# A delta rule and two expert layers: weight groups of the second layer split in another order, a second output buffer, waits by accumulator

## The reference

```python
for t in range(S):
    y[:, :, t] = einsum('bhd,bhde->bhe', q[:, :, t], state)
    v_old = einsum('bhde,bhd->bhe', state, k_n[:, :, t])
    state = state + beta_t * outer(k_n[:, :, t], v_t - v_old)
h = x @ w_in            # first layer
g = where(h >= 1, h, where(h <= -1, 0, (h + 1)**2 / 4))
x = g @ w_out
h = x @ w_in2           # second layer
r = maximum(h, 0.0)
out = (r * r) @ w_out2
```

## Time and profile before

| | |
|---|---|
| median of three runs | 1002.56 us (1001.31 to 1002.76) |
| profiled execution | 1000.11 us, its span 998.0 us |
| mean granted clock of TensorE | 0.975 of full speed |
| PE (TensorE matmul) busy | 951.9 us, 95% |
| VectorE (DVE), ScalarE (ACT), GpSimd (POOL) busy | 669.7, 455.0, 171.4 us |
| longest waits of PE | 14.9, 5.1, and two of 1.9 us |

### The profile page before, as it was taken

The page is one execution under the profiler, slowest core; times in us unless marked ns, Lnnn a source line. Parts: engine busy times, 40 slices in busy tenths (PEclk is TensorE's granted clock), DMA queues, the critical chain, the costliest instruction groups (busy, mean ns, idle before and its releaser), DMA issues. The chain is left out here.

```text
span 998.0 us, 23043 instructions
## 1 busy us (share of the span) xinstructions
PE 951.9 (95%) x9448; PEld 768.6 (77%) x9448; DVE 669.7 (67%) x1566; ACT 455.0 (46%) x768; POOL 171.4 (17%) x165
## 2 busy tenths in 40 slices
PE   7899999999999999999999965999999999999997
PEld 6688788778777877787788854788877888878885
DVE  7789789787888888797545424655656565646553
ACT  6667443554454445435445433433543334533333
POOL 5810000000000000000025855560223001400000
PEclk7799999999999999999999996999999999999999
DMA  7252140122012101200030321210011000010001
GB/s 252 82 171 65 59 129 34 34 71 73 18 34 88 56 17 34 60 33 2 12 133 5 107 68 38 75 63 2 0 60 68 1 1 1 22 41 1 1 1 64
DMA packets 31015, 51.71 MB, mean 52 GB/s; under 512 B 2496, under 2 KB 19904, under 8 KB 30912
## 3 DMA queue, kind: packets, MB, share of 16 engines
q1 hardware_dynamic: 30912, 50.24, 15.2%
HBM read 40.80 MB, written 9.44 MB: 50 GB/s over the span
## 5 line engine op out<-in xcount | busy, mean ns | idle before, releaser
L1555 PE MATMUL psum<-x_high,w 128*128 128x512 f32 x528 | 193.1, 396 | 21.5 <-DVE act_g L2038 16.4
L1546 PE MATMUL psum<-g_hi,w 128*128 128x512 f32 x576 | 197.6, 399 | 0.0
L1527 PE MATMUL psum<-x_hi,w 128*128 128x512 f32 x576 | 197.3, 398 | 0.0
L2003 DVE TENSOR_TENSOR act_g<-act_g 128x512 f32<-128x512 f32 x96 | 74.4, 775 | 97.6 <-ACT act_g L1126 68.2
L1555 PEld LDWEIGHTS psum<-x_high,w 128*128 128x128 f32 x528 | 100.6, 191 | 45.7 <-issue 22.8
L1546 PEld LDWEIGHTS psum<-g_hi,w 128*128 128x128 f32 x576 | 108.4, 188 | 26.3 <-issue 2.0
L1527 PEld LDWEIGHTS psum<-x_hi,w 128*128 128x128 f32 x576 | 108.0, 188 | 26.4
L1546 PE MATMUL psum<-g_lo,w 128*128 128x512 f32 x288 | 112.5, 391 | 0.0
L1527 PE MATMUL psum<-x_lo,w 128*128 128x512 f32 x288 | 111.9, 390 | 0.0
L1034 ACT ACTIVATE act_g<-act_g,half 128x512 f32<-128x512 f32 x86 | 62.1, 723 | 106.1 <-DVE act_g L1955 105.6
L1625 PE MATMUL psum<-quad_hi,w 128*128 128x512 f32 x288 | 105.8, 395 | 3.8 <-ACT y_out L1060 3.8
(11 more groups left out here) (187 smaller groups left out, 1448.9 us busy)
## 6 DMA issues: line engine op xcount, KB each, us to landing
kt_sb<-in_k_t SPq DMA_DIRECT2D x24, 256.0 KB, 4.1
qt_sb<-in_q_t SPq DMA_DIRECT2D x23, 256.0 KB, 3.3
ring<-in_v_s SPq DMA_DIRECT2D x24, 192.0 KB, 2.9
between_layers<-y_out SPq DMA_DIRECT2D x6, 768.0 KB, 4.0
x_raw<-between_layers SPq DMA_DIRECT2D x6, 768.0 KB, 5.7
result<-y_out SPq DMA_DIRECT2D x5, 768.0 KB, 3.4
gram_or_states<-in_k_s SPq DMA_DIRECT2D x15, 192.0 KB, 2.4
x_raw<-in_w_in SPq DMA_DIRECT2D x6, 384.0 KB, 3.0
```

The source lines that it names most:

```text
L1527: ins = pe.matmul(h_ps[n % 2][:, :], w_in_part(f // GW, part)[:, kt, fs], x[:, kt, :], start=(at == 0), stop=(at == len(terms) - 1))
L1546: ins = pe.matmul(acc_ps[0][kt][:, :], w_out_part(f // GW, part)[:, f % GW, ds], g[n % 2][:, :], start=(f == 0 and j == 0), stop=(f == NF ...
L1555: ins = pe.matmul(bank[at][:, :], weight[:, part, w * P:(w + 1) * P], moving[:, x, :], start=(first and c == 0 and j == 0), stop=(c == len ...
L2003: dve.tensor_tensor(quad_act(b)[:, :], quad_act(b)[:, :], quad_act(b)[:, :], ALU.mult).then_inc(square_ready, 1)
```

## The change

Six things are changed.

- `stage2_of`: groups 0 and 1 go through `early_stage`, groups 2 to 7 through `x2_raw`. The waits in `load_weights2` follow that.
- The order: POOL combines and splits group 0 between the sums and the low parts of the inputs; ACT splits groups 0, 1, 2 in steps 2, 8 and 11 of the last tile, and 3, 4, 5, 6, 7 in quads 0, 1, 2, 4 and 5, at four different places of the quad. `x2_part` waits for the sum that it reads and no longer for all five.
- `first_quad`: the second product of step 95 is cut in its three row blocks, laid ahead of `t_products`, `c00_product` and `c10_products`; `u_product(1)` comes behind two block outputs and no longer ahead of them.
- `out_of`: odd tiles are drained to `x2_sum[:, 0:3, :]`, even ones to `y_out`; two semaphores `out2_stored` count the stores.
- `block_output` of a new pair waits for the one accumulator that it writes.
- `x2_sums` of the last pair is spread over quads 10 to 14, one sum behind each `part_w`.

```diff
--- before.py
+++ after.py
@@ -194,7 +194,7 @@
 
         def stage2_of(g):
 
-            return (0, g // 2 + 1) if g in (0, 2) else (1, {1: 1}.get(g, g - 1))
+            return (0, g + 1) if g < 2 else (1, g - 1)
 
         def staged2(g):
 
@@ -214,6 +214,10 @@
         def free_for_w2(g):
 
             return (0, 1, 2, 3, 5, 6, 7)[g]
+
+        def out_of(t):
+
+            return x2_sum[:, 0:KT, :] if t % 2 else y_out[:, :, :]
 
         def x2_source(i):
 
@@ -377,6 +381,7 @@
 
         ws_loaded = [sem(f"ws_loaded{i}") for i in range(3)]
         w2_loaded = [sem(f"w2_loaded{i}") for i in range(2)]
+        out2_stored = [sem(f"out2_stored{i}") for i in range(2)]
         w2_combined = sem("w2_combined")
         w2_hi_ready = sem("w2_hi_ready")
         w2_lo_ready = sem("w2_lo_ready")
@@ -628,10 +633,10 @@
 
             def load_weights2(g):
                 at = stage2_of(g)[0]
-                if g == 1:
+                if g == 2:
                     sp.wait_ge(x2_lo_ready, X_COMBOS)
                 elif g:
-                    sp.wait_ge(w2_lo_ready, 2 * (g - 1 if g in (2, 3) else g))
+                    sp.wait_ge(w2_lo_ready, 2 * g)
                 cols = slice(g * GW * P, (g + 1) * GW * P)
                 sp.dma_start(plain_in(g).rearrange("p k f m -> p k (f m)"), w_in2.rearrange("(k p) f -> p k f", p=P)[:, :, cols]
                              ).then_inc(w2_loaded[at], 16)
@@ -664,7 +669,7 @@
 
             def store_out(t):
                 sp.wait_ge(acc_ready, KT * (NTT + t + 1))
-                sp.dma_start(out.rearrange("(k p) (t j) -> t p k j", p=P, j=TT)[t], y_out[:, :, :]).then_inc(out_stored, 16)
+                sp.dma_start(out.rearrange("(k p) (t j) -> t p k j", p=P, j=TT)[t], out_of(t)).then_inc(out2_stored[t % 2], 16)
 
             for m in range(B):
                 load_kt(m)
@@ -746,9 +751,10 @@
                 store_out(t)
             for kt in range(KT):
                 sp.wait_ge(acc_ready, KT * (2 * NTT - 1) + kt + 1)
-                sp.dma_start(out.rearrange("(k p) (t j) -> t p k j", p=P, j=TT)[NTT - 1][:, kt, :], y_out[:, kt, :]
-                             ).then_inc(out_stored, 16)
-            sp.wait_ge(out_stored, 16 * (2 * NTT - 1 + KT))
+                sp.dma_start(out.rearrange("(k p) (t j) -> t p k j", p=P, j=TT)[NTT - 1][:, kt, :], out_of(NTT - 1)[:, kt, :]
+                             ).then_inc(out2_stored[1], 16)
+            sp.wait_ge(out2_stored[0], 16 * TOK_PAIRS)
+            sp.wait_ge(out2_stored[1], 16 * (TOK_PAIRS - 1 + KT))
 
 
         @block.gpsimd
@@ -782,9 +788,13 @@
 
                 pool.wait_ge(raw_loaded, 32 * (pair + 1))
                 wait(pool, x2_lo_ready, X_COMBOS * pair)
+                if pair > 1:
+                    pool.wait_ge(out2_stored[1], 16 * (pair - 1))
                 for i, (n, k), (n2, k2), op in ((0, (1, 0), (0, 1), ALU.subtract), (1, (1, 0), (1, 1), ALU.add),
                                                 (2, (0, 0), (1, 0), ALU.add), (3, (0, 0), (0, 1), ALU.add),
                                                 (4, (0, 1), (1, 1), ALU.add)):
+                    if pair > 1:
+                        pool.wait_ge(w_part_ready, NG * (pair - 1) + i + 3)
                     pool.tensor_tensor(x2_sum[:, i, :], x2_raw[:, n, k, :], x2_raw[:, n2, k2, :], op).then_inc(x2_sum_ready, 1)
 
             def x2_lows(pair):
@@ -864,8 +874,10 @@
                     pool.wait_ge(ds_done, BY_BLOCK * B)
                     pool.memset(u_rows, 0.0).then_inc(u_rows_zero, 1)
             x2_sums(0)
+            combine_weights(0)
+            low_weights(0)
             x2_lows(0)
-            for g in range(NG):
+            for g in range(1, NG):
                 combine_weights(g)
                 low_weights(g)
             for pair in range(1, TOK_PAIRS):
@@ -996,7 +1008,7 @@
             def x2_part(pair, i):
 
                 act.wait_ge(raw_loaded, 32 * (pair + 1))
-                act.wait_ge(x2_sum_ready, X_SUMS * (pair + 1))
+                act.wait_ge(x2_sum_ready, X_SUMS * pair + (1, 1, 2, 3, 3, 3, 4, 4, 5)[i])
                 if pair:
                     last_of = (u_done, w_done, c11_done, t_part_done, c00_done, c10_done, c10_done, c01_done, c01_done)[i]
                     act.wait_ge(last_of, NG * pair)
@@ -1050,14 +1062,19 @@
                     act.activation(y_out[:, kt, :], acc_ps[0][kt][:, :], ACT.Copy).then_inc(acc_ready, 1)
 
             def drain2(pair, tok):
-                act.wait_ge(out_stored, 16 * (NTT + 2 * pair + tok))
+                if pair:
+                    act.wait_ge(out2_stored[tok], 16 * pair)
+                elif tok == 0:
+                    act.wait_ge(out_stored, 16 * NTT)
+                if tok:
+                    act.wait_ge(x2_lo_ready, X_COMBOS * min(pair + 2, TOK_PAIRS))
                 last = pair == TOK_PAIRS - 1 and tok == 1
                 if not last:
                     act.wait_ge(block_done, blocks_by(NG * (pair + 1) - 1, 3 if tok else 2))
                 for kt in range(KT):
                     if last:
                         act.wait_ge(tail_done, kt + 1)
-                    act.activation(y_out[:, kt, :], acc2_of(pair, tok)[kt][:, :], ACT.Copy).then_inc(acc_ready, 1)
+                    act.activation(out_of(tok)[:, kt, :], acc2_of(pair, tok)[kt][:, :], ACT.Copy).then_inc(acc_ready, 1)
 
             def block_high(q, b):
                 act.wait_ge(square_ready, blocks_by(q, b))
@@ -1100,8 +1117,8 @@
                     if 3 <= f < 8:
                         for i in range(2 * (f - 3), min(2 * (f - 2), X_COMBOS)):
                             x2_part(0, i)
-                    if f in (8, 11, 13, 15):
-                        high_weights((8, 11, 13, 15).index(f))
+                    if f in (2, 8, 11):
+                        high_weights((2, 8, 11).index(f))
 
             def quad(q):
                 pair, g = divmod(q, NG)
@@ -1111,7 +1128,7 @@
                 act.wait_ge(u_done, q + 1)
                 wait(act, w_part_ready, q)
                 if q == 0:
-                    act.wait_ge(w2_lo_ready, 6)
+                    act.wait_ge(w2_lo_ready, 4)
                 act.activation(part_u[:, :], bank[0][:, :], ACT.Copy).then_inc(u_part_ready, 1)
                 if g == 1 and pair:
                     drain2(pair - 1, 1)
@@ -1130,13 +1147,15 @@
                 if following:
                     x2_part(following, 2)
                     x2_part(following, 3)
-                if q < 4:
-                    high_weights(q + 4)
+                if q in (0, 4):
+                    high_weights(6 if q else 3)
                 act.wait_ge(c00_ready, q + 1)
                 block_relu(1)
                 if following:
                     x2_part(following, 4)
                 block_high(q, 1)
+                if q == 5:
+                    high_weights(7)
                 act.wait_ge(c10_ready, q + 1)
                 block_relu(2)
                 if following:
@@ -1145,11 +1164,15 @@
                 block_high(q, 2)
                 if g == 0 and pair:
                     drain2(pair - 1, 0)
+                if q == 1:
+                    high_weights(4)
                 act.wait_ge(c01_ready, q + 1)
                 block_relu(3)
                 if following:
                     x2_part(following, 7)
                     x2_part(following, 8)
+                if q == 2:
+                    high_weights(5)
 
             act.wait_ge(half_ready, 1)
             act.activation(norm_t[:, 0, 0:1], half[:, 0:1], ACT.Sqrt).then_inc(root_table, 1)
@@ -1528,7 +1551,7 @@
                                     start=(at == 0), stop=(at == len(terms) - 1))
                 ins.then_inc(h_done, 1)
 
-            def second_product(n):
+            def second_product(n, parts=tuple(range(KT))):
                 t, f = divmod(n, NF)
                 if t == 0 and f % GW == 0:
                     pe.wait_ge(w_hi_ready, 2 * (f // GW) + 2)
@@ -1540,12 +1563,13 @@
                         pe.wait_ge(x_lo_ready, B)
                     else:
                         pe.wait_ge(acc_ready, KT * t)
-                for kt in range(KT):
+                for kt in parts:
                     ds = slice(kt * P, (kt + 1) * P)
                     for j, (part, g) in enumerate(((HIGH, g_hi), (HIGH, g_lo), (LOW, g_hi))):
                         ins = pe.matmul(acc_ps[0][kt][:, :], w_out_part(f // GW, part)[:, f % GW, ds], g[n % 2][:, :],
                                         start=(f == 0 and j == 0), stop=(f == NF - 1 and j == 2))
-                ins.then_inc(mm2_done, 1)
+                if KT - 1 in parts:
+                    ins.then_inc(mm2_done, 1)
 
             def combined(q, at, pairs, first):
 
@@ -1618,8 +1642,8 @@
                     if b == 0 and q == 0:
                         pe.wait_ge(x_ready, ITEMS - B)
                         pe.wait_ge(kq_ready, 2 * ITEMS)
-                    elif b < 2 and g == 0:
```

(12 more changed lines are left out.)

## The result

The changed kernel takes 976.9 us (median of 4 runs, 975.94 to 977.68) against 1001.93 for the kernel before beside it: a ratio of 0.9755, 95% interval 0.9731 to 0.978. It was timed twice more, at 977.1 and 977.5. The forecast was 978.3 with a range of 970 to 988.

What follows compares the result with a forecast made beforehand. PE was taken as busy 951.9 of 998.0 us, its remaining waits mostly at the layer handover and drains. Gains 16.8 - 1.6 + 1.1 + 5.9 + 2.1 = 24.3 took 1002.56 to 978.3 us, range 970 to 988.

Steps and rivals of the forecast that it cites:

- Order of the groups: Handover between layers: group 3 ready near 578, stop ahead of c11 0 (bound 0.4), gain 5.22 + 1.68 us.
- First quad: Quad 0: stops of 2.4 ahead of c01, 3.2 ahead of `u_product(1)`, slow clock 2.2; handover loses 7.8, gains 16.8 us.
- Groups 4 to 7: Later quads, splits through one stage and sums of pair 1: 2.65 us lost against 1.05, loss 1.6 (gain 1 to loss 4).
- Sums of pair 2: Sums spread behind `part_w`: the 1.1 us stop at 760.92 goes, gain 1.1 us.
- Drains: Changes of pair: both PE stops for a drain and the slow stretch go, gain 5.9 us (bounds 4 and 5.9).
- End: Last drain and stores: last drain's end 3.5 us earlier, span's end gains 2.1 us (bounds 1.5 and 3.4).
- the half-shut handover: Rival, handover: late ACT step paid in full, clock falls twice or group 5 misses its slot; 984 us, chance 0.22.
- The slower one: Rival, quads 1 and 2: a single-stage round doesn't fit between slots, each ACT hold costs 17.7; 1014 us, chance 0.03.

Runs made afterwards that it cites:

- the run with group 3 late: Changed kernel with group 3's split on ACT moved from ahead of relu(1) of quad 0 to behind relu(3): 976.61 us, ratio 0.9771 to the kernel before.

## Why the prediction was right

*Order of the groups.* Forecast a stop of 0 ahead of c11 with a bound of 0.4; measured 0. Forecast group 3 combined near 578; POOL ended at 577.0. The hold in step 2 cost nothing.

*First quad.* Forecast stops of 2.4 and 3.2 and 2.2 of slow clock, 7.8; measured 2.4, 4.0 and 2.84, 9.25 in all, and 8.15 in the two later traces. The drain to c00 took 584.75 to 587.48, 2.73 as taken from the earlier trace rows. The term that was too small is the chain from the square to `c01_ready`: 589.28 to 594.99, 5.7 us for 4.75. Its first instruction took 2.29 us beside POOL's low part and not the 1.29 of the earlier trace rows; the bound of 4.5 for the stop held it. The row for it stood in the trace of the kernel before. There the split of group 4 was directly ahead of relu(1) in quad 1, as the split of group 3 now is in quad 0, and the same square took 2.23:

```profile
605.36 2.23 DVE L2003 TENSOR_TENSOR act_g<-act_g 128x512 f32<-128x512 f32 x1 [10.81 <-ACT act_g L1068]
...
610.34 0.67 DVE L2038 TENSOR_TENSOR act_g<-part_w,psum 128x512 f32<-128x512 f32 x1
```

From this square to the end of the subtraction it is 5.65 us. With that in place of 4.75 the forecast of the stop would have been 4.1.

*Groups 4 to 7.* Forecast 2.65 lost in place of 1.05. Measured 5.2 in place of 1.3, the weakest step, still within its bound of 4 (3.9). Three sizes were off. Group 4's split was said to have 2.6 us to spare; 0.84 were lost, since square(3) beside POOL took 2.29 (613.61) and moved `block_high(3)` and `part_u` by that. Group 7's stop was 2.3 and not 1.3, for the same reason (2.27 at 675.41), and 1.7 of slow clock behind it hadn't been counted. And the sums of pair 1 cost nothing where 1.0 was taken: at 685.75 to 693.4 they meet squares of 1.15 and 0.97, but not the two that end the chain.

*Sums of pair 2.* Forecast 1.1, measured 1.2. Each takes 1.29 directly behind a `part_w` (746.57, then every 15.6 us).

*Drains.* Forecast 5.9, measured 5.85; the two halves were each shown alone.

*End.* Forecast 2.1, measured 1.6. The stores ran at 416, 401 and 387 GB/s in the windows above, for 414 assumed, and the last one landed 1.95 us behind the first, for 1.9. The rest of the miss is behind that landing: 0.76 us to the end of the span, for 0.40 in the kernel before. The Trainium skill, page "DMA: Bandwidth & Descriptors", section "Where 436 GB/s comes from", has the HBM side bind at about 358 GB/s for one core: these windows disagree. The estimate of 1.5 for the gain that was made with it is nearer to the measured one than mine all the same, by luck, since the bytes did not take the time that it gives them.

The errors had both signs (handover -1.1, groups -2.3, sums +0.1, end -0.5, start of the second layer +1.4, which nothing in the forecast stands for). The sum was 24.3 for 22.1 between the profiled spans, and 25.0 between the medians; part of that nearness is luck, since the median before moves by 2.8 us between groups of runs.

Of the rivals, the half-shut handover came in small: its late step as a stop of 4.0 for 3.2, and its second fall of the clock, where one was forecast, not in the profiled execution but in both later traces, where the first of the two lay inside the wait and cost nothing (the last section). Group 5 met its slot, and the price of 984 was not reached. The slower one, a round that misses its slot, is real as a mechanism: it decided the run with group 3 late. In the changed kernel it didn't occur, group 5 being combined at 626.2 for its slot at 628.50.

## What to carry to other kernels

When one stage feeds several weight groups, write down the round (high part, low part, load, combination: here 15 us) and look for a place in the consumer's order where that engine idles and the next critical result is far: between `part_u` and relu(0), not ahead of a relu whose square ends the chain. Work that is cut to fill an idle queue must not be what another engine drains ahead of a critical step. Price an instruction beside a contending engine by how much of the other engine's instruction is left when it starts, from a row with the same order of work just ahead of it; here a row with 0.74 us left was taken for a place with 1.75 left.

## What the runs showed of the hardware

*A slow clock inside a wait is free.* In two executions of the same kernel 6.83 us passed from the start of c01 to `u_product(1)` of the handover (588.31 to 595.14, and 590.43 to 597.26), though the clock differed. In the first trace it held through the block outputs and fell only at 594.3, in the second wait; 14 matmuls behind 595.14 were slow (2.84 lost, the windows above). In the next one it fell at about 590.7, right behind the 2.2 us stop, so that c01 and the block outputs were slow, and returned before the wait ended; a second slow stretch was shorter (1.67 lost):

```profile
590.00:591.00 1.00, 0.57 (x2) 0.83 1.08 455
...
593.00:594.00 1.00, 1.00 (x4) 0.50 0.00 0
...
595.00:596.00 1.00, 0.00 (x1) 1.00 0.00 0
...
597.00:598.00 1.00, 0.74 (x2) 0.75 0.96 299
...
601.00:602.00 1.00, 1.00 (x6) 1.00 0.00 0
```

The chain on ACT and DVE set the end of the wait in both. A stop's price in slow clock thus varies: none behind the stops of 1.0 and 1.2 us at the pair changes, 1.7 behind one stop of 2.1 there in the kernel before and none behind the other, 1.7 behind the 2.3 of u(6) but none in the run with group 3 late, and 1.7 to 2.8 at the handover.

*Beside POOL.* A DVE instruction with two inputs in SBUF that starts while an instruction of POOL's low part runs ends 0.55 us behind the end of that instruction, however much of it is left. For the square at 589.28 it is this one, which ends at 591.03 (the square at 591.58):

```profile
588.08 2.95 POOL L825 TENSOR_TENSOR w<-x_raw,w 128x1280 fp32r<-128x1280 f32 x1 [11.11 <-ACT w L1027]
```

In the second layer's part of the fourteen traces there are 127 such instructions, with 0.18 to 1.79 us left on POOL. All end 0.55 or 0.56 behind it, so they took 0.73 to 2.33 us in place of 0.69. The 1.29 of the earlier trace rows had 0.74 left. One with an input in PSUM kept 0.67 to 0.69 (591.50, inside the low part's second instruction, and 677.61). The Trainium skill, page "GPSIMD Engine Reference", section "8. Key points", says that GpSimd contends with VectorE instructions that have two SBUF inputs; the traces agree, with 2.33 for 0.69 at the worst.
